# Sums of squares on ScalarE for the weight scales, one cast per group, and another order of the sums and the weight pieces

## The reference, cut to what matters

```
x = attention(q, k, v, w_phi)                 # 2304 rows x 512
P = sinkhorn(exp(x @ w_gate), 8 rounds)       # 2304 x 8
for e in range(8):                            # "dense" layer, the subject here
    h = max(x @ w1[e], 0)                     # 512 -> 1024
    out += P[:, e:e+1] * (h @ w2[e])          # 1024 -> 512
then each row goes to the expert of its largest logit, same shapes of weights
```

## Time and profile before

| | |
|---|---|
| median of 2 runs | 2353.06 us (2352.75 to 2353.37) |
| the profiled execution | 2346.36 us, span of the profile 2344.5 us |
| mean granted TensorE clock | 0.951 |
| PE, DVE, ACT, POOL busy | 86%, 70%, 38%, 21% of the span |

### The profile page before, as it was taken

How to read it: one execution, slowest core, us unless ns; L and a number is a source line. 1 busy time by engine, 2 the same in 40 slices (tenths; PEclk the granted TensorE clock), 3 DMA queues, 4 the chain that set the end, 5 groups by cost and what they waited for, 6 DMA issues and landing times.

```text
span 2344.5 us, 45908 instructions
## 1 busy us (share of the span) xinstructions
PE 2024.1 (86%) x17514; PEld 1696.6 (72%) x17514; DVE 1646.7 (70%) x3287; ACT 893.0 (38%) x1755; POOL 481.2 (21%) x310
## 2 busy tenths in 40 slices
PE   6968978789689878979987898889789999699998
PEld 5757867677568767867776687778677888566765
DVE  7847887788677777777767767877777775734343
ACT  3535433334334344434433343443344443222221
POOL 0633842300320230041004102300410000111211
PEclk9979979899899989999998999999999999889999
DMA  6132021224222132313312231323132322261420
GB/s 189 36 92 62 21 73 45 73 91 164 71 108 100 46 108 91 136 64 109 109 65 91 100 118 46 112 88 136 63 109 77 116 106 82 95 265 42 177 97 11
DMA packets 123162, 221.73 MB, mean 95 GB/s; under 512 B 63542, under 2 KB 63670, under 8 KB 121792
## 3 DMA queue, kind: packets, MB, share of 16 engines
q1 hardware_dynamic: 111888, 183.62, 22.9%
q10 hardware_dynamic: 7056, 25.69, 3.2%
q0 software_dynamic: 4000, 9.45, 1.3%
HBM read 151.88 MB, written 70.52 MB: 95 GB/s over the span
## 4 chain that ended last, share of the span: by engine, by line
PE 53%; DVE 23%; issue 11%; ACT 5%; DMA 4%; POOL 3%; SPq 0%; DVEq 0%; ACTq 0%; POOLq 0%
PE ps L950 17%; PE ps L927 16%; PE ps L1111 6%; DVE arena L1556 4%; PE ps L1095 4%; DVE wg L1414 4%; DVE arena L1631 3%; PE ps L876 3%; DVE arena L1568 2%; DMA arena<-in_moe_w_dram 2%; DVE arena L1559 2%; PE ps L1097 2%; DVE arena L1558 2%; PE ps L889 2%; ACT arena L1193 2%
## 5 line engine op out<-in xcount | busy, mean ns | idle before, releaser
L950 PE MATMUL ps<-arena 128*128 128x256 f16 x6048 | 769.9, 281 | 214.1 <-DVE arena L1631 197.7
L950 PEld LDWEIGHTS ps<-arena 128*128 128x128 f16 x6048 | 595.6, 101 | 340.4 <-DVE arena L1631 211.0
L927 PE MATMUL ps<-arena 128*128 128x256 f16 x6912 | 808.3, 273 | 5.7 <-ACT arena L1231 5.1
L927 PEld LDWEIGHTS ps<-arena 128*128 128x128 f16 x6912 | 677.8, 98 | 87.2 <-ACT arena L1231 6.4
L1231 ACT ACTIVATE arena<-ps 128x256 f32<-128x256 f32 x576 | 206.9, 377 | 574.1 <-PE ps L927 563.0
L1568 DVE TENSOR_TENSOR arena<-arena 128x384 f16<-128x384 f32 x576 | 383.8, 667 | 4.3 <-ACT arena L1238 3.5
L1240 ACT ACTIVATE arena<-arena 128x512 f16<-128x512 f32 x288 | 181.4, 630 | 426.1 <-DVE arena L1561 426.1
L1631 DVE SCALAR_TENSOR_TENSOR arena<-ps,wt,arena 128x256 f32<-128x256 f32 x441 | 211.5, 480 | 155.3 <-PE ps L950 152.8
L1556 DVE TENSOR_TENSOR arena<-arena 128x128 f32<-128x128 f32 x288 | 142.0, 493 | 190.2 <-ACT arena L1231 189.2
L602 POOL PARTITION_ALL_REDUCE wm<-wg x32 | 12.2, 380 | 816.9 <-DVE wg L1414 766.6
L720 POOL TENSOR_TENSOR arena<-arena 128x1024 f16<-128x1024 f32 x49 | 106.9, 2186 | 312.3 <-ACT arena L1180 305.2
(11 more groups left out here) (213 smaller groups left out, 1893.8 us busy)
## 6 DMA issues: line engine op xcount, KB each, us to landing
arena<-in_moe_w_dram SPq DMA_DIRECT2D x16, 2048.0 KB, 9.0
split_weights<-arena SPq DMA_DIRECT2D x64, 512.0 KB, 3.0
arena<-in_moe_w_dram SPq DMA_DIRECT2D x64, 512.0 KB, 4.9
arena<-split_weights SPq DMA_DIRECT2D x8, 4096.0 KB, 13.6
second_weights<-arena SPq DMA_DIRECT2D x49, 512.0 KB, 3.2
arena<-second_weights ACTq DMA_DIRECT2D x49, 512.0 KB, 3.7
arena<-in_q_dram SPq DMA_DIRECT2D x16, 288.0 KB, 3.6
arena<-in_k_dram SPq DMA_DIRECT2D x16, 288.0 KB, 4.0
```

What stands on the lines that cost most here:

```text
L927: last = pe.matmul(o, ring[:, slot, sw, FF * c + 128 * j:FF * c + 128 * j + 128], xT[:, sx, c, BLK * blk:BLK * blk + BLK], start=(i == 0), ...
L950: last = pe.matmul(region(n, u), hop[:, u, sh, p, o, :], w2op[:, o, sw, p, :], start=(i == 0 and k in (0, 1, 3)), stop=(i == 3 * Q - 1), s ...
```

## The change

VectorE's `largest` stays for the first two weights (in the attention); for the other 30 the reduction becomes ScalarE's Square with a sum over the row (`bound`), two quarters at a point, and the scale is made from half the exponent. GpSimd's instruction stays and waits for these sums. In groups 0 to 2 the two casts of ScalarE become one of seven operands behind the sums, and the two low-part instructions of VectorE one of seven; group 3 keeps two of each. In VectorE's queue the sums come ahead of the weight work: scale, sums, `accumulate`, low parts, then Sinkhorn's step and the low parts of weights. In ScalarE's queue the weight work of groups 0 to 2 now stands between the relus and the cast; in group 3 it stays behind it. The table `PLANS` is the same.

```
@@ tensor scale on GpSimd
-                        across(wm[:, u, :], wg[:, u, :], RMAX, wmax_done, n + 1, wall_done)
+                        across(wm[:, u, :], wg[:, u, :], RMAX, bound_done, WP * (n - 1), wall_done)
@@ TensorE
-                    pe.wait_ge(hlo_done, FC * (ub + 1) - 1)
+                    pe.wait_ge(hlo_done, HALVES * (ub + 1) - 1)
@@ ScalarE
-                act.activation(hop[:, u, 0, p, 0:3, :], tb[:, p % 2, 0:3, :], ACT.Copy).then_inc(hhi_done, 1)
+                o0 = 0
+                if p == Q - 1:
+                    act.activation(hop[:, u, 0, p, 0:3, :], tb[:, p % 2, 0:3, :], ACT.Copy).then_inc(hhi_done, 1)
+                    o0 = 3
                 act.wait_ge(hsum_done, 4 * (Q * ub + p + 1))
-                act.activation(hop[:, u, 0, p, 3:OPS, :], tb[:, p % 2, 3:OPS, :], ACT.Copy).then_inc(hhi_done, 1)
+                act.activation(hop[:, u, 0, p, o0:OPS, :], tb[:, p % 2, o0:OPS, :], ACT.Copy).then_inc(hhi_done, 1)
+
+            def bound(plan, par, e, job, k):
+                n = number(plan, e, job)
+                done, value = loads(plan, e, job)
+                u = PLANS[plan]["order"].index(job) % 2
+                if k == 0:
+                    act.wait_ge(done, 16 * value)
+                    act.wait_ge(wall_done, n - 1)
+                seen = WP * (n - 2) + k - 1
+                if due(seen):
+                    act.wait_ge(bound_done, seen)
+                act.activation(spent[:, k % 2, :], raw_of(plan, par, job)[:, WPC * k:WPC * k + WPC], ACT.Square,
+                               accum_out=wg[:, u, k:k + 1]).then_inc(bound_done, 1)
+
+            def weights_hook(plan, c, par, e, h):
+                if h in PLANS[plan]["top"]:
+                    job, k0 = PLANS[plan]["top"][h]
+                    for k in (k0, k0 + 1):
+                        bound(plan, par, e, job, k)
+                for job, k in PLANS[plan]["hi"].get(h, ()):
+                    cut_hi(plan, c, par, e, job, k)
...
+                            if p < Q - 1:
+                                weights_hook(plan, c, par, e, Q * blk + p)
                             operands_hi(ub + 1, (par + blk + 1) % 2, p)
...
-                            for job, k in PLANS[plan]["hi"].get(Q * blk + p, ()):
-                                cut_hi(plan, c, par, e, job, k)
+                            if p == Q - 1:
+                                weights_hook(plan, c, par, e, Q * blk + p)
@@ VectorE, the scale from a sum of squares
+                bits = inv.bitcast(i32)
+                dve.tensor_scalar(bits, wsc[:, at, 0:1].bitcast(i32), 1, EXPMASK, ALU.arith_shift_right, ALU.bitwise_and)\
+                   .then_inc(wscale_done, 1)
...
+                dve.tensor_scalar(inv, inv, 2.0 ** (64 - TOP), 2.0 ** -(56 + TOP), ALU.mult, ALU.max).then_inc(wscale_done, 1)
...
+                dve.reciprocal(wsc[:, at, 3:4], inv).then_inc(wscale_done, 1)
@@ VectorE, the order in a block
                         for p in range(Q):
+                            scale_hook(plan, par, e, Q * blk + p)
+                            operand_sums(ub + 1, p)
+                            if p == Q - 1:
+                                operands_lo(ub + 1, 1 - u, p, 0)
+                            accumulate(e, blk, ub, p + 1, plan, u)
+                            operands_lo(ub + 1, 1 - u, p, 1 if p == Q - 1 else None)
+                            if p == Q - 1:
+                                accumulate(e, blk, ub, 5, plan, u)
+                                accumulate(e, blk, ub, 6, plan, u)
                             if plan == "first":
                                 sinkhorn(Q * blk + p)
                             weights_hook(plan, c, par, e, Q * blk + p)
...
-                            operand_sums(ub + 1, p)
-                            operands_lo(ub + 1, 1 - u, p, 0)
-                            accumulate(e, blk, ub, p + 1, plan, u)
-                            operands_lo(ub + 1, 1 - u, p, 1)
-                        for k in (5, 6):
-                            accumulate(e, blk, ub, k, plan, u)
```

More of the change, by code:

```diff
@@ L106, in moe_attention_kernel @@
         stage = view(O_STAGE, 2 * 2 * WPC, f16).rearrange("p (u s n) -> p u s n", u=2, s=2)
+        spent = view(ARENA - 4 * WPC, 2 * WPC, f16).rearrange("p (u n) -> p u n", u=2)
         hbuf_f = view(O_STAGE, D, f32)
@@ L1227, in relu_rows @@
                 act.wait_ge(h1_done, FC * ub + n + 1)
-                if x == 0 and due(FC * ub + n - 2):
-                    act.wait_ge(hlo_done, FC * ub + n - 2)
+                if x == 0:
+                    read = HALVES * ub + p - 1 if p > 1 else HALVES * (ub - 1) + 3 + 2 * p
+                    if due(read):
+                        act.wait_ge(hlo_done, read)
                 dst = tb[:, p % 2, 1:3, :] if x else tb[:, p % 2, 0:S3 + 1:S3, :]
@@ L1422, in weight_scale @@
                 dve.wait_ge(wscale_done, 4 * n + 1)
-                scale_of(wscale_done, 4 * n + 1, wsc[:, at, 0:1], wsc[:, at, 3:4], inv)
+                if isinstance(n, int) and n < 2:
+                    scale_of(wscale_done, 4 * n + 1, wsc[:, at, 0:1], wsc[:, at, 3:4], inv)
+                    return
+                bits = inv.bitcast(i32)
+                dve.tensor_scalar(bits, wsc[:, at, 0:1].bitcast(i32), 1, EXPMASK, ALU.arith_shift_right, ALU.bitwise_and)\
+                   .then_inc(wscale_done, 1)
+                dve.wait_ge(wscale_done, 4 * n + 2)
+                dve.tensor_scalar(inv, inv, 2.0 ** (64 - TOP), 2.0 ** -(56 + TOP), ALU.mult, ALU.max).then_inc(wscale_done, 1)
+                dve.wait_ge(wscale_done, 4 * n + 3)
+                dve.reciprocal(wsc[:, at, 3:4], inv).then_inc(wscale_done, 1)
+                dve.wait_ge(wscale_done, 4 * n + 4)
             def cut_lo(plan, c, par, e, job, k):
@@ L1434, in cut_lo, with scale_hook @@
                                          in1=hi, op0=ALU.mult, op1=ALU.subtract).then_inc(wlo_done, 1)
-            def weights_hook(plan, c, par, e, h):
-                if plan == "second" and h == 0:
-                    cut_lo("first", 0, 0, 0, "B1", WP - 1)
-                if h in PLANS[plan]["top"]:
-                    job, k0 = PLANS[plan]["top"][h]
-                    done, value = loads(plan, e, job)
-                    u = PLANS[plan]["order"].index(job) % 2
-                    for k in (k0, k0 + 1):
-                        largest(number(plan, e, job), u, raw_of(plan, par, job), k, done, value)
+            def scale_hook(plan, par, e, h):
                 if h in PLANS[plan]["scale"]:
@@ L1457, in weights_hook @@
                                           inv, 1.0, None, ALU.mult)
+            def weights_hook(plan, c, par, e, h):
+                if plan == "second" and h == 0:
+                    cut_lo("first", 0, 0, 0, "B1", WP - 1)
                 for job, k in PLANS[plan]["lo"].get(h, ()):
@@ L1561, in operand_sums, with operands_lo @@
                 dve.tensor_tensor(t[:, S4, :], t[:, A12, :], t[:, S2, :], ALU.subtract).then_inc(hsum_done, 1)
-            def operands_lo(ub, u, p, x):
-                some = slice(0, 3) if x == 0 else slice(3, OPS)
-                dve.wait_ge(hhi_done, FC * ub + 2 * p + x + 1)
-                if x == 1:
+            def operands_lo(ub, u, p, x=None):
+                some = slice(0, OPS) if x is None else slice(0, 3) if x == 0 else slice(3, OPS)
+                dve.wait_ge(hhi_done, HALVES * ub + p + 1 + (x or 0))
+                if x != 0:
                     dve.wait_ge(hsum_done, 4 * (Q * ub + p + 1))
@@ L1770, in _ @@
                 operand_sums(0, p)
-                operands_lo(0, 0, p, 0)
-                operands_lo(0, 0, p, 1)
+                if p == Q - 1:
+                    operands_lo(0, 0, p, 0)
+                operands_lo(0, 0, p, 1 if p == Q - 1 else None)
                 if p == 0:
```

5 lines of the change are left out of this document (3 added, 2 removed).

## The result

The changed kernel takes 2519.98 us (median of 2 runs, 2516.80 to 2523.16) against 2353.06: ratio 1.0709, 95% interval 1.0651 to 1.0768. Its profiled execution is the one of 2523.16 us, 176.8 above the one of before. It is slower, as forecast; the median is 40 above the predicted one and inside the range.

A forecast was written before the change was run, and what follows sets the result against it. Bound: TensorE's waits for VectorE's `accumulate`, without reserve at product 6. Five "rest" experts at +18 (+90), second +18, first +20, last -1: +127 on 2346.4 gives 2473 profiled, 2480 us median; range 2335 to 2555.

The forecast's parts named there:

- Slot wait, block 2: "Rest" experts, block 2: B0-1's cut waits for B0-0's slot, holding the cast; +5 us (bounds -3, +8).
- Slot wait, block 3: "Rest" experts, block 3: the same wait with S3, S4, B0-2, B0-3, no GpSimd chain; +5 us (1 to 7).
- Block 1: "Rest" experts: later squares delay GpSimd's scaling; S0, at 17.4, holds group 2's cast; +2.7 us.
- Block 5: "Rest" experts: maxima at points 20 and 21 leave VectorE, group 3's sums start at 18.2; -2 us.
- block 4: "Rest" experts: squares at 17 and 18, S5 and S6 at 17 delay group 1's cast; +2.5 us (0 to 3.3).
- Block 7: "Rest" experts: A's pieces at points 0 and 1, 5.0 against 2.2 of slack; +4 us with the slower clock.
- First and second expert: Second: slot waits and A's pieces, +18 us; first: slot waits and later GpSimd sums behind Sinkhorn's step, +20 us.
- Last: The last expert, with neither S nor A: -1 us.
- Rival (a): Slot waits hide behind GpSimd's chain; about +3 us an expert, +15 for the first two; 2383 us; chance 0.17.
- the longer group: VectorE's group takes 3.2 us instead of 2.6, waiting for one cast; slack for weight work 2.2 instead of 4.0.
- Rival (b): Faster: VectorE's relief decides, group 3's sums come on time; put at 2290 us; chance 0.11.
- Rival (c): Square needs table loads, two of 1.28 a pair: 154 us more on ScalarE, up to 2630; chance 0.04.

The follow-up runs named there:

- run 2: Changed kernel with Sinkhorn's step and the low pieces ahead of the sums again on VectorE: 2454.1 us, 1.0472.
- Run 7: Changed kernel with both old orders (ScalarE's cuts behind the cast, VectorE's low pieces ahead of the sums), squares and one cast kept: 2441.3 us, 1.0402.
- run 6: Kernel before with only the casts and low parts of groups 0 to 2 merged into one instruction each: 2432.8 us, 1.0382.
- run 3: Changed kernel with two casts and two low parts a group again in groups 0 to 2: 2485.0 us, 1.0606.
- run 10: Squares behind two casts, low pieces ahead of sums (group 3: behind last accumulate), product 0's wait relaxed, S's low parts moved from GpSimd to VectorE: 2255.1 us, 0.9615.
- run 1: Changed kernel with ScalarE's high parts behind the cast again in groups 0 to 2, squares still ahead of it: 2452.5 us, 1.0467.
- run 12: Run 10 with B0's second pair of squares and the high and low parts of S5 and S6 moved to other points: 2232.7 us, 0.9509.

## Why the prediction was right, and where its sizes were off

**The frame held.** Product 6 is where a block ends late, the three that wait 8.5 us or more run at the lower of the two clocks (2.74 instead of 1.47; granted clock 0.50), the one of block 7, which waits 2.21, partly so (2.33; 0.60), and the terms add up by block. Against the profiled execution +127 was forecast and +177 came (+167 between the medians).

**Slot wait, block 2.** By the steps: B0-1 at offset 18.1 (measured 1835.69 - 1817.64 = 18.05), S2 at 20.5 (21.6), sums of group 3 at 24.8 (25.7), product 6 4 to 8 behind (8.4). The chain of waits was right, and two sizes in it were not. S1's DMA was put at 4.4 and took 5.7 (issued at 1833.53, S2 cut at 1839.24). And product 6 followed the sums by more than the 4 to 8 allowed; +5 was taken from inside that range, and +8.1 came. The two bounds of this term do not follow from its steps either: 24.8 + 8 is 32.8, 6.7 behind the 26.05 of before and not 8, and sums at 24.8 without a collision put product 6 at 26.8, not at 22. That the result met the +8 is therefore no proof of the sum. The group was late enough to meet L722 and all of GpSimd's sums, which is no chance event, since the same high part S2 that delays the cast starts them.

**Slot wait, block 3.** +7.6 against +5 (1 to 7), outside its bounds. What I had missed stands in group 0: S3 too waits for a DMA, 1.92, since B0-1's low piece (end of block 2) goes out just ahead of S2 in SyncE's queue. So group 1 is late too: B0-2's low piece ends at offset 16.2, where B0-0's ended at 14.9 in block 2, B0-3 is cut at 19.4 instead of 18.1 and S4 at 22.9 instead of 20.5, S3's DMA being slower than 4.4 as well. Blocks 2 and 3 together were short by 5.7 us an expert, 28 over five, of the 50 that were missing.

**Block 1.** S0 was forecast at offset 17.4 and came at 17.3; +3.8 against +2.7. **Block 5** -3.0 against -2, **block 4** +2.2 against +2.5, **block 6** +1.0 against +0.8, **block 0** -0.3 against 0. **Block 7**: the sums of groups 1, 2 and 3 were put at 11.0, 16.5 and 19.6. VectorE there (block start 1956.11):

```profile
1963.57 1.09 DVE L1604 TENSOR_TENSOR arena<-arena 128x896 f16<-128x896 f32 x1 [1.37 <-ACT arena L1247]
...
1966.97 0.29 DVE L1592 TENSOR_TENSOR arena<-arena 128x128 f32<-128x128 f32 x1
...
1972.59 0.28 DVE L1592 TENSOR_TENSOR arena<-arena 128x128 f32<-128x128 f32 x1
...
1975.81 0.28 DVE L1592 TENSOR_TENSOR arena<-arena 128x128 f32<-128x128 f32 x1
```

10.9, 16.5 and 19.7: +4.2 against +4. With the low pieces ahead of the sums (run 2) it is 21.6 long, 1 from a free block.

**First and second expert**: 38 forecast, 47 measured; they hold slot waits too, but were not followed block by block. **Last**: -1 forecast, +5 measured for all that follows; not looked into.

**Rival (a)** was mispriced. It said that without the slot waits +3 an expert would be left, 1.013. Run 7 has the longer group and the squares, no wait of B0's or B1's high parts and no late pieces of A, so it should have been cheaper still, and it is 1.040. The mis-sized term is the longer group: the rival gives it and A's pieces about +3 an expert, and run 6 shows 87 us of it alone. The error hid in the forecast as well: there, the longer group was inside blocks whose end the slot wait set anyway, and on top of the rest it costs 1.0 point (run 3). That the total came out inside the range owes something to this overlap, which the prediction did not work out; that is luck. The prediction's own figures (3.2 a group against 2.6) gave it, had I put them through blocks 0 to 5 of an expert without a slot wait. **Rival (b)**, VectorE's relief: its busy time fell by 157 us (about 150 forecast), and no run shows a gain from that. **Rival (c)**: no table load was added; see below.

**Unsettled.** What the two orders cost without the squares, and how the 3% of run 10 divide. The first two experts were not followed block by block.

## What to carry to other kernels

Ahead of an instruction that a whole chain waits for, put nothing that can wait for a DMA, and count what stands behind it up to the next such instruction (runs 1 and 12); when two reorderings are made at once, follow one buffer through both, since an earlier writer and a later reader cost little alone (up to 0.7 points each, against 3.1 together). Judge a move to an idle engine by the time that it has free in the one interval where it is wanted, not by its share of the span: here 2.0 us in each 3.93. Merging two instructions saves a little on each engine (one cast 0.95 instead of 0.52 + 0.63) and serialises what was overlapped; here, where the consumer is the critical engine, the overlap was worth 3.8%.
